# One padded token stream in 7 units of 440 columns, instead of 8 units of 384, in a fused attention, convolution-gated and channel-mix kernel

## The reference

```python
# attention with a decaying state, 8 heads of 48 channels
for t in range(S):
    cur = einsum('bhd,bhe->bhde', u * kt, vt)
    y[:, :, t] = einsum('bhd,bhde->bhe', rt, state + cur)
    state = w * state + einsum('bhd,bhe->bhde', kt, vt)
# 384 channels -> 1024 -> 384, convolution over three tokens, gate
h = maximum(x @ w_in, 0)
conv_out = sum_k conv_w[k] * h shifted by k - 1 (zeros beyond each batch's ends)
x = (h * sigmoid(conv_out)) @ w_out
# layer norm over channels, 384 -> 1536 -> 384, residual
xn = (x - mean) / sqrt(var + 1e-6) * g_ln
out = x + maximum(xn @ w_ch1, 0) @ w_ch2
```

## Time and profile before

| | us |
|---|---|
| median of 3 runs | 712.81 (709.88 to 713.77) |
| profiled execution, its own time | 707.88 |
| its span, first to last instruction | 706.1 |
| PE busy in the span | 667.2 (94%) |
| PEld busy | 658.5 (93%) |
| DVE busy | 418.5 (59%) |
| ACT busy | 224.8 (32%) |
| POOL busy | 110.3 (16%) |
| mean granted PE clock | 0.973 |

### The profile page before, as it was taken

How to read it: one execution, slowest core, us unless ns; L and a number is a source line. 1 busy time by engine, 2 the same in 40 slices (tenths; PEclk the granted TensorE clock), 3 DMA queues, 4 the chain that set the end, 5 groups by cost and what they waited for, 6 DMA issues and landing times.

```text
span 706.1 us, 11248 instructions
## 1 busy us (share of the span) xinstructions
PE 667.2 (94%) x4116; PEld 658.5 (93%) x4116; DVE 418.5 (59%) x787; ACT 224.8 (32%) x440; POOL 110.3 (16%) x131
## 2 busy tenths in 40 slices
PE   3888889999999999999999999999999999999798
PEld 3878889999999989999999999999999998999798
DVE  7869964388624964369724785259653684128412
ACT  0565221154212621144311542126311542117311
POOL 4631031201221031110312002210311101000100
PEclk9979979999999999999999999999999998999999
DMA  8960102201202012020122022020120200000000
GB/s 229 369 194 11 57 1 57 67 25 56 57 1 91 24 35 57 23 69 24 34 57 68 24 57 57 1 90 22 34 57 24 67 1 1 1 34 0 1 1 33
DMA packets 15632, 37.21 MB, mean 53 GB/s; under 512 B 2528, under 2 KB 8928, under 8 KB 15584
## 3 DMA queue, kind: packets, MB, share of 16 engines
q1 hardware_dynamic: 15584, 36.53, 17.0%
HBM read 31.80 MB, written 4.72 MB: 52 GB/s over the span
## 4 chain that ended last, share of the span: by engine, by line
PE 44%; issue 37%; DVE 10%; POOL 6%; ACT 2%; POOLq 0%; DVEq 0%
PE hid L365 7%; PE hid L367 6%; PE hid L366 6%; PE acc L365 5%; PE acc L367 5%; PE acc L366 5%; PE att_ps L378 2%; PE att_ps L410 2%; POOL rstd L836 2%; POOL raw_n L816 1%; POOL raw_n L818 1%; PE att_ps L406 1%; POOL raw_n L831 1%; DVE a_sb L709 1%; DVE xn L738 1%
## 5 line engine op out<-in xcount | busy, mean ns | idle before, releaser
L365 PE MATMUL acc<-w_hi,ring_hi 128*128 128x384 f32 x480 | 163.3, 340 | 0.4 <-ACT ring_hi L517 0.4
L366 PE MATMUL acc<-w_lo,ring_hi 128*128 128x384 f32 x480 | 161.7, 337 | 0.0
L367 PE MATMUL acc<-w_hi,ring_lo 128*128 128x384 f32 x480 | 161.6, 337 | 0.0
L750 DVE SCALAR_TENSOR_TENSOR ring_lo<-hid,ring_hi 128x384 fp32r<-128x384 f32 x96 | 53.5, 557 | 162.1 <-ACT ring_hi L563 162.0
L563 ACT ACTIVATE ring_hi<-hid 128x384 fp32r<-128x384 f32 x96 | 47.2, 492 | 256.8 <-PE hid L367 256.8
L365 PE MATMUL hid<-xnt_hi,w_hi 128*128 128x384 f32 x288 | 103.8, 361 | 1.3 <-DVE xnt_lo L744 1.3
L367 PE MATMUL hid<-xnt_hi,w_lo 128*128 128x384 f32 x288 | 99.3, 345 | 0.0
L366 PE MATMUL hid<-xnt_lo,w_hi 128*128 128x384 f32 x288 | 99.1, 344 | 0.0
L365 PEld LDWEIGHTS acc<-w_hi,ring_hi 128*128 128x128 f32 x480 | 90.1, 188 | 1.3 <-issue 1.0
L366 PEld LDWEIGHTS acc<-w_lo,ring_hi 128*128 128x128 f32 x480 | 90.1, 188 | 0.0
L367 PEld LDWEIGHTS acc<-w_hi,ring_lo 128*128 128x128 f32 x480 | 90.0, 188 | 0.0
(11 more groups left out here) (123 smaller groups left out, 989.9 us busy)
## 6 DMA issues: line engine op xcount, KB each, us to landing
raw_t<-rk_t SPq DMA_DIRECT2D x44, 192.0 KB, 3.2
raw_n<-rk_n SPq DMA_DIRECT2D x22, 384.0 KB, 3.6
w_raw<-weights SPq DMA_DIRECT2D x10, 768.0 KB, 12.4
out<-x SPq DMA_DIRECT2D x24, 192.0 KB, 1.9
v_sb<-v_n SPq DMA_DIRECT2D x22, 192.0 KB, 2.4
first_raw_t<-rk_t SPq DMA_DIRECT2D x4, 192.0 KB, 7.3
first_raw_n<-rk_n SPq DMA_DIRECT2D x2, 384.0 KB, 10.3
first_v<-v_n SPq DMA_DIRECT2D x2, 192.0 KB, 10.3
```

The source lines that it names most:

```text
L365: mm(ps, lh, rh, start=start and n == 0, stop=False)
L366: mm(ps, lh, rl, start=False, stop=False)
L367: last = mm(ps, ll, rh, start=False, stop=stop and n == len(terms) - 1)
L750: stt(ring_lo[:, tile % RING, :], hid[f % 2][:, 0:UT], 0.0, f32_of(ring_hi[:, tile % RING, :]), ALU.max, ALU.subtract).then_inc(dve_fl, 1)
```

## The change

- **Units.** The four batches lie one after the other in one stream of columns, a zero column between two batches. It is cut into 7 units of 440 output columns (the last 436), two more for the convolution. Chunks are placed by `places(m)`, so that a chunk may be split over two units, and units take 3, 4, 3, 4, 3, 3 and 0 chunks of attention. `xt_hi` and `xt_lo` are doubled.
- **Second products.** `second` now has the weights as stationary operand and 440 tokens as columns, so its result is channels-first.
- **Layer norm.** The means over channels are taken out of `w_ch1` once (`column_means`, `column_mean`, `centre`), so `ffn1` works on `x2` as it is. The transposes, `stats` and `xn` are gone. The sums over channels are made by POOL (`sums`) and a product with ones (`total`), twice a unit; `variance` adds epsilon, POOL raises 440 columns to the power -0.5 (`rstd`), and `scaled` multiplies the second product by it before `result`.
- **Attention.** `scores` multiplies 48 rows at partitions 0 and 64 instead of 112 rows with zeros between; `kv` has 48 stationary columns and writes partitions 0 and 64; `kd` is written over `k`; `scale` is one DVE operation instead of three; `rk` is double-buffered and loaded by one DMA.
- **Order.** All 7 units are written out; no loop. The lists are new.

```diff
-UT = S // 2
-TT = UT // P
+WIDTH = 440
+UNITS = 7
+N_OF = [WIDTH] * 6 + [436]
+PADS = {0: (0, 1), 1: (329, 1), 3: (218, 1), 5: (107, 1), 6: (436, 2)}
...
 PE_PLAN = [
...
-    ("norm", 0), ("kv", 1), ("norm", 1), ("norm", 2), ("y", 1, 1), ("part", 0, 3), ("xt", 1),
-    ("ffn1", 2), ("ffn2", 0), ("ffn1", 3), ("ffn2", 1), ("scores", 2, 0),
...
+    ("mm2", 4), ("scores", 1), ("mm2", 5), ("xt", 0), ("mm2", 6, 7), ("y", 1),
+    ("ffn1", 0), ("kv", 1), ("ffn1", 1), ("xt", 1), ("ffn1", 2), ("ffn2", 0), ("ffn1", 3), ("ffn2", 1), ("total", 0),
+    ("ffn1", 4), ("ffn2", 2), ("scores", 2), ("ffn1", 5), ("ffn2", 3), ("ffn1", 6), ("total", 1), ("ffn2", 4),
+    ("ffn1", 7), ("ffn2", 5), ("y", 2), ("kv", 2), ("ffn1", 8), ("ffn2", 6), ("xt", 2), ("ffn1", 9), ("scores", 3),
+    ("ffn2", 7), ("ffn1", 10), ("ffn2", 8), ("y", 3), ("kv", 3), ("ffn1", 11), ("ffn2", 9), ("xt", 3), ("ffn2", 10, 11)]
...
 DVE_PLAN = [
...
+    ("x2_low", 0), ("x2_low", 1), ("x2_low", 2), ("w_low", 5), ("flow", 0), ("centre", 1), ("x_sum", 1), ("flow", 1),
...
+    ("off_mean", 0), ("off_mean", 1), ("flow", 4), ("off_mean", 2), ("centre", 2), ("flow", 5),
+    ("variance",), ("masked", 2, 0), ("masked", 2, 1), ("w_low", 8), ("dots", 2), ("flow", 6), ("w_low", 9), ("flow", 7),
...
+    ("scaled", 0), ("scaled", 1), ("result", 0), ("scaled", 2), ("result", 1), ("result", 2)]
 POOL_PLAN = [
...
+    ("pad",), ("ruk", 0), ("kd", 0), ("cv", 0), ("sums", 0), ("ruk", 1), ("kd", 1), ("cv", 1), ("sums", 1),
+    ("ruk", 2), ("kd", 2), ("rstd",), ("cv", 2), ("ruk", 3), ("kd", 3), ("cv", 3)]
...
+                for hp in range(NP):
+                    for q in range(2):
+                        rows = slice(64 * q, 64 * q + D)
+                        last = mm(banks_of(m)[q][:, hp * P:(hp + 1) * P], rk_of(m)[rows, 1, hp, :],
+                                  rk_of(m)[rows, 0, hp, :], start=True, stop=True)
...
+                        last = mm(banks_of(m)[3][64 * q:64 * q + D, hp * D:(hp + 1) * D], raw_n_of(m)[:, 1, cols],
+                                  v_of(m)[:, cols], start=True, stop=True)
...
+                if tiles[0] == 0:
+                    if layer == 1:
+                        pe.wait_ge(act_x2, KT * u + KT)
+                    elif u:
+                        pe.wait_ge(dve_out, KT * u)
+                    else:
+                        pe.wait_ge(act_cm, KT)
+                for k in range(KT):
                     for f in tiles:
...
+                        last = split_product(acc[k][:, 0:n], w_hi[:, cols], w_lo[:, cols],
+                                             ring_hi[:, slot, 0:n], ring_lo[:, slot, 0:n], f == 0, f == end - 1)
...
+            def total(u, i):
...
+                mm(att_ps[2][:, 0:n], one[:, 0:1].to_broadcast([P, P]), row_sum[:, 0:n],
+                   start=True, stop=True).then_inc(pe_sum, 1)
...
+            def column_means():
...
+                for j in range(KT):
...
+                    for k in range(KT):
+                        at_k = PIECE_AT[f"c1_{j}"] + k * 512
+                        last = mm(acc[j][:, :], mean_g[:, k, :], w_raw[:, at_k:at_k + 512],
+                                  start=k == 0, stop=k == KT - 1)
...
+            def scale(m):
...
+                x = rk_of(m)[0:ROWS, :, :, :].rearrange("p a h t -> p (a h t)")
+                tt(x, x, powrk[0:ROWS, :, :, :].rearrange("p a h t -> p (a h t)"), ALU.mult).then_inc(dve_rk, 1)
...
+            def x2_low(u, k):
...
+                dve.wait_ge(act_xhi, KT * u + k + 1)
+                tt(x2_lo[:, k, 0:n], acc[k][:, 0:n], f32_of(x2_hi[:, k, 0:n]), ALU.subtract).then_inc(dve_x2l, 1)
...
+            def variance(u):
...
+                nc.vector.tensor_scalar(row_sum[:, 0:n], att_ps[2][:, 0:n], EPS, None, ALU.add).then_inc(dve_var, 1)
...
+            def scaled(u, k):
...
+                acc_whole(dve, u, 1, k)
+                dve.wait_ge(pool_rs, u + 1)
+                tt(acc[k][:, 0:n], acc[k][:, 0:n], row_sum[:, 0:n], ALU.mult).then_inc(dve_scaled, 1)
...
+            def sums(u, i):
...
+                tt(o, a, b, ALU.add).then_inc(pool_half, 1)
...
+                tt(row_sum[:, 0:n], o, c, ALU.add).then_inc(pool_sum, 1)
...
+            def rstd(u):
...
+                tt(row_sum[:, 0:n], row_sum[:, 0:n], nhalf[:, 0:1].to_broadcast([P, n]), ALU.pow).then_inc(pool_rs, 1)
```

More of the change, by code:

```diff
@@ new lines, in places @@
+def places(m):
+    a, found = chunk_start(m), []
+    for w in range(UNITS):
+        first, end = max(a, WIDTH * w), min(a + P, WIDTH * w + N_OF[w] + 2)
+        if first < end:
+            found.append((w, first - WIDTH * w, first - a, end - a))
+    return found
+LAST = [max(m for m in range(CHUNKS) if any(w == u for w, *_ in places(m))) for u in range(UNITS)]
+CHUNKS_IN = [range(LAST[u] + 1, LAST[u + 1] + 1) for u in range(UNITS - 1)] + [range(0)]
+THIRD = {c[2]: u for u, c in enumerate(CHUNKS_IN) if len(c) > 2}
@@ L72 @@
-    ("fhi", 6), ("fhi", 7), ("fhi", 8), ("fhi", 9), ("fhi", 10), ("xh", 2), ("fhi", 11)]
-DVE_PLAN = [
[L74 to L86, removed]
@@ L93, with each_unit @@
 OF_STATE = {"kv", "state", "kd"}
[L94 to L111, removed]
+OF_FIRST = {"table", "column_means", "column_mean", "w_hi", "w_low", "centre"}
+def each_unit(plan, do):
+    for u in range(UNITS):
+        for kind, *a in plan:
+            if kind in OF_FIRST:
+                if u == 0:
+                    do[kind](*a)
+            elif kind not in ATTENTION:
+                do[kind](u, *a)
+            elif a[0] < len(CHUNKS_IN[u]):
+                m = CHUNKS_IN[u][a[0]] + LATER.get(kind, 0)
+                if m < CHUNKS and not (kind in OF_STATE and m % CH == CH - 1):
+                    do[kind](m, *a[1:])
 def states_made(m):
@@ L495, in _ @@
             last.then_inc(pe_tab, 1)
-            pe.wait_ge(dve_set, 3)
-            scores(0, 0, 0)
-            scores(0, 0, 1)
-            kv(0, 0)
-            scores(0, 1, 0)
-            scores(0, 1, 1)
+            pe.wait_ge(dve_set, 2)
+            scores(0)
+            kv(0)
+            scores(1)
             for m in range(AHEAD):
-                y(0, m, 0)
-                y(0, m, 1)
+                y(m)
                 if m + 1 < AHEAD:
-                    kv(0, m + 1)
-                for half in range(2 if m + 2 < AHEAD else 0):
-                    scores(0, m + 2, half)
-                xt(0, m)
-            each_unit(pe, PE_PLAN, {
-                "scores": scores, "kv": kv, "y": y, "xt": xt, "mm1": mm1, "ffn1": ffn1, "part": part, "norm": norm,
-                "mm2": lambda b, g, *f: second(b, g, 0, *f), "ffn2": lambda b, g, *f: second(b, g, 1, *f)})
+                    kv(m + 1)
+                if m + 2 < AHEAD:
+                    scores(m + 2)
+                xt(m)
+            each_unit(PE_PLAN, {
+                "scores": scores, "kv": kv, "y": y, "xt": xt, "mm1": mm1, "ffn1": ffn1, "total": total,
+                "column_means": column_means,
+                "mm2": lambda u, *f: second(u, 0, *f), "ffn2": lambda u, *f: second(u, 1, *f)})
         @block.scalar
@@ new lines, in square @@
+            def square(u, k):
+                d = dev[k][:, 0:N_OF[u]]
+                act.wait_ge(dve_dev, KT * u + k + 1)
+                nc.scalar.activation(d, d, ACT.Square, scale=DM ** -0.5).then_inc(act_sq, 1)
+            act.wait_ge(pool_set, 1)
+            for m in range(AHEAD):
+                if m:
+                    w_high(m - 1)
+                xh(m)
+            act.wait_ge(ld_cw, 32)
+            for k in range(KT):
+                last = copy(mean_g[:, k, :], part[:, 0:1].to_broadcast([P, P]), scale=gl[:, k:k + 1])
@@ L759, in _, with result @@
+            def result(u, k):
+                n = N_OF[u]
+                dve.wait_ge(dve_scaled, KT * u + k + 1)
+                tt(x2[:, k, 0:n], acc[k][:, 0:n], x2[:, k, 0:n], ALU.add).then_inc(dve_out, 1)
+            scale(0)
             dve.wait_ge(pe_tab, 1)
```

834 lines of the change are left out of this document (410 added, 424 removed), and 9 rows, old and new, of the table PE_PLAN.

## The result

| | before | after |
|---|---|---|
| median, us | 711.35 (707.12 to 713.77, 4 runs) | 1020.4 (1018.93 to 1022.43, 4 runs) |
| ratio to before | | 1.436, 95% interval 1.428 to 1.443 |
| profiled span, us | 706.1 | 1018.6 |
| PE, DVE, ACT, POOL busy, us | 667, 419, 225, 110 | 671, 388, 228, 619 |
| mean granted PE clock | 0.973 | 0.833 |

The four runs of before are the three on record ahead of the prediction and one more. The forecast was 688 us. The change made the kernel 309 us slower, and rival 3 of the prediction (POOL's power), chance 0.13, is what happened.

A forecast was written before the change was run, and what follows sets the result against it. PE, 94% busy, was taken as the bound. From the span of 706.1 us, -4.6 - 27 + 18 - 5 - 8 + 1 + 1 gave 681.5, scaled to a median of 688 us; own range 672 to 700, overall 668 to 714.

The forecast's parts named there:

- rival 3: The power on POOL becomes the bound: 800 us at 0.1 us a column, over 2,000 at 0.55; chance 0.13.
- POOL's power: Power of 440 columns in rstd: between 0.95 and 242 us, taken as hidden within about 28 us of slack.
- Wider units: Split matmuls of 440 columns instead of 384, 199.4 ns each if overhead is per matmul: -4.6 us (-5 to +1.5).
- The norm: Norm between the two products: 32 us of stalls and transposes go, 5 us left in their place: -27 us (-30 to -15).
- Added products: New PE products of total (10.3 us) and column_means (7.7 us), not hidden: +18 us (+9 to +19).
- Tiles: Tiled attention scores and kv: half the possible scores saving, nothing for kv, 4 us for switches: -5 us (-28 to +44).
- Rival 2: Tile switches eat the attention's saving: 715 us without overlap at 0.25 us a switch; bad form 708 to 720, chance 0.12.
- Start-up: Before the first dense matmul: less DVE work brings it from 47.0 to about 39 us: -8 us (-13 to 0).
- Unit 0: First unit, with weight splits and centre on DVE and ACT: 2 us lost, loop turn gone: +1 us (-2 to +8).
- Rival 4: The stall only moves: DVE's list or first mm2's wait holds PE 2 to 3 us a unit: 705 us, chance 0.15.

The follow-up runs named there:

- f1: Kernel with the root on ACT, a chunk's scores products issued four at rows 0, then four at rows 64, not in turns: 697.64 us, ratio 0.983.
- f3: Kernel with the root on ACT, the 8 kv products of every chunk made twice in a row: 690.90 us, ratio 0.975.
- g1: Kernel with the root on ACT, kv products made twice only in the four chunks ahead of the first unit: 685.20 us, ratio 0.961.
- g3: Kernel with the root on ACT, start-up kv doubled, four products of ones added early, first unit's second centre moved later on DVE: 682.45 us, ratio 0.960.

## Why the prediction was wrong, step by step

**The step that failed** is "POOL's power": "28 us would be 64 ns a column, 29 times that. I take the hidden case, since most of the 0.55 us for a single column can be what every call costs." Measured, a column costs 160 ns and a call 0.25 us, so the call takes 70.5 us and 48 of them show. The bounds were right (0.95 to 242 us). The slack was put somewhat high as well, 28 us where 22 to 23 were measured; that is 6 of the 48. The value was taken near the low end by comparison with POOL's other operations, which says nothing of a power. The rows named did not decide between the bounds: the 2.2 ns a column of a product was itself worked out with nothing fixed. The trace of before had a hint that was not used, POOL's smallest cheap calls:

```profile
L808 POOL MEMSET one<- 128x2 f32 x1 | 0.1, 100 | 0.0
```

If a call costs no more than these 0.10 us, some 0.45 of the 0.55 are the column's own, an estimate of 198 us for 440. A memset is not a power, so this gives no value, but it speaks against a hidden one. The range should have held it.

**Rival 3** was right in its mechanism and its point of decision. At 160 ns a column its own sum gives 688 + 7 x (70.5 - 28) = 985.5; the measured 1020.4 is 35 more: 7 x 5.7 us of slack put too high, 40, less the 4.5 us by which the base was lower.

**The other terms**, read from the kernels without the power. Their sum was to take 24.6 us from the span of 706.1; the run with the product has a span of 681.1, 25.0 less. That they agree so well is luck: the start-up (8 us), unit 0 (some 5) and the width (1.6) came out worse than taken, the tiles (8) and the norm (5) better.

- *Wider units: right.* PE's timeline with ACT's root, which answers to the earlier trace rows; 16 starts apart:

```profile
178.16 0.36 PE L352 MATMUL acc<-ring_lo,w_hi 128*128 128x440 f32 x1
...
181.36 0.36 PE L353 MATMUL acc<-ring_hi,w_lo 128*128 128x440 f32 x1
```

  3.20 us for 16 starts, 200 ns, against 199.4 foretold and 201.8 if the 16 ns were per column. The gain is 2520 x 0.200 against 2880 x 0.1761, 3 us.
- *The norm: right, and better.* Of the 5 us that were left in its place next to nothing came. With ACT's root, y's last records and the first ffn1 of a unit follow each other without idle time at full clock; these answer to the earlier trace rows:

```profile
190.76 0.57 PE L400 MATMUL att_ps<-v_sb,att 128*128 128x48 f32 x4
191.15 0.44 PE L351 MATMUL hid<-x_hi,w_hi 128*128 128x440 f32 x1
```

- *Added products: right.* +10.4 measured for 14 more `total`; the records of the column means are 0.43 us apart.
- *Tiles: better than taken.* The scores saved what was taken, 9.5 us. Each of their two halves stood like this before, with the eight records of the earlier trace rows between the two lines:

```profile
248.95 0.34 PE L367 MATMUL acc<-w_hi,ring_lo 128*128 128x384 f32 x1
...
250.19 0.34 PE L366 MATMUL acc<-w_lo,ring_hi 128*128 128x384 f32 x1
```

  From the product before to the second one after, less two products, a half costs 1.24 - 0.35 = 0.89 us. The 16 records of now cost 230.82 - 229.13 - 0.40 = 1.29. So a chunk saves 0.49 us, 20 chunks 9.8, and only the paired order brings it (f1). By the same count kv went from 0.89 to 0.70 us, 3 us in 16 chunks, where a switch cost of 4 us was taken and no gain. Both counts have the changes of tiling in them. For these by themselves: before the 16 kv records (the lines shown with f3) PE passes from whole to 48 columns. The four of y take 0.39 us when the next work is dense (190.76 to 191.15), and 0.50 there (238.22 to 238.72), so 0.1 more. In scores, 229.13 + 0.20 to 229.42 is 0.09 us. On the way back the first dense product takes 0.31 us instead of 0.20 (230.51 to 230.82), where it took 0.25 instead of 0.18 before without a change of tiling. So the rule of the Trainium skill (TensorEngine Tiling (Array Packing), Tiling Modes, Key Properties), a drain at a change of tiling, costs here about 0.1 us a switch and not the 0.32 of the bound. Rival 2 is out. Of the same page's up to 2x for a dimension of at most 64 the scores' paired records reach 1.5 (1.64 us to the next product without the pairs, 1.09 with them).
- *Start-up: missed.* -8 was taken, nothing came (first dense product at 46.7 to 47.7 without doubled kv, against 47.0). DVE did get its relief, and PE became what was late. The window of the start-up with the changed kernel answers to the earlier trace rows; below it are a piece of its last third, a piece of PE's timeline there, and the same piece of the kernel before:

```profile
9.00:47.00 38.00, 33.44 (x228) 31.20 (x228) 23.85 (x38) 8.03 (x12) 18.99 (x19) 1.00 1.03 317
30.00:41.00 11.00, 11.00 (x72) 10.59 (x73) 7.80 (x13) 3.56 (x4) 1.47 (x2) 1.00 1.02 345
```

```profile
39.43 0.98 PE L399 MATMUL acc<-first_v,first_att 128*128 128x48 f32 x4
40.21 0.71 PE L395 MATMUL acc<-state,first_rk 112*128 112x96 f32 x2
```

```profile
40.62 0.57 PE L410 MATMUL acc<-first_v,first_att 128*128 128x48 f32 x4
41.03 0.43 PE L406 MATMUL acc<-state,first_rs 112*128 112x96 f32 x2
```

  DVE is busy 23.9 of 38 us instead of 31.7, PE 33.4 instead of 29.7, and from 30 to 41 us all the time. The columns of its products are the same as before, but four records of y take 40.21 - 39.43 = 0.78 us where the same four took 41.03 - 40.62 = 0.41 us before, about the ratio of the two clocks. f3 is the test: with PE fast from 18.8 us to 33.8 its first dense product came at 41.5, under the same share of the DMAs (1.03). The Trainium skill (TensorE: Matmul & The Clock Gate, Part 1) has the low clock as the state that activity ends; the traces don't decide it here, since PE in g1, with the same instructions as f3, became fast some 23 us later. Why the kernel before was fast in this stretch and the changed one was not stays open.

- *Unit 0: missed as well.* +1 was taken. PE's waits with ACT's root show two that are new:

```profile
PE att_ps L407 <- DVE raw_n L707: 3.7, 1, 3.7
PE acc L351 <- ACT col_mean L519: 2.9, 1, 2.9
```

  The first is `centre` in DVE's list, 1.3 us an operation there, where 0.6 would follow from `w_low`'s 1.8 us for 1536 columns; g3 took it away. The second is PE waiting for the column means, which ACT copies out of the accumulators; no run tried to move it.

Rival 4 (the stall only moves) is out outside unit 0: no wait of PE for DVE or ACT there is longer than 1.3 us.

## What to carry to other kernels

Price the transcendental or power operation of an engine per element from the smallest call there is, and take the call's fixed cost from a cheap operation on the same engine; then ask how many columns the new call has. A value that is the same on all partitions should not be computed on a wide row: with the tokens on the partitions the same power is 50 times cheaper (1.4 us instead of 70.5 a unit), and ACT does the root of the wide row in 0.57 us after a table load of 1.28. Where a late result sits in front of an in-order list, the waits name the neighbours: follow the chain to the one instruction that is long.

## What the runs showed of the hardware that was not expected

- A power on POOL costs 0.25 us and 160 ns a column of 128 partitions, linear from 160 to 440 columns (25.83, 41.82, 70.47 us), and 0.55 and 0.86 us for one and three columns, against 0.92 us for 440 columns of a product.
- fp32 products of 48 rows at partitions 0 and 64, in turns: 16 records in 1.16 us; the same with the four of each half together: 1.71.
- In the start-up the changed kernel's small products ran at the lower clock (0.20 us a record of y against 0.10 before), although the windows print a clock of 1.00 there: the distances of the starts decide, not the printed clock. In f3 the records were fast from 18.8 to 33.8 us, in g1, with the same instructions, from about 42 us. What makes the speed rise in one execution and not in another is open.
- `centre` on DVE took 0.7 us for 512 columns while POOL was idle, and 1.3 and 1.5 us while POOL was busy, with ACT's root; POOL's operations beside it took 1.3 to 1.5 us where 1.0 to 1.1 is their time elsewhere. The three calls of three operations each:

```profile
78.84 2.07 DVE L651 SCALAR_TENSOR_TENSOR w_raw<-w_raw,gl,col_mean 128x512 f32<-128x512 f32 x3
102.02 3.79 DVE L651 SCALAR_TENSOR_TENSOR w_raw<-w_raw,gl,col_mean 128x512 f32<-128x512 f32 x3
119.69 4.54 DVE L651 SCALAR_TENSOR_TENSOR w_raw<-w_raw,gl,col_mean 128x512 f32<-128x512 f32 x3
```

  They go together in this trace; no run moved one and left the other.
